# Expert loop of an attention and mixture-of-experts kernel: x and h transposed together, each iteration ending on layer 2, the last tile taken out of the loop

## The reference, cut to what matters

```python
# attention: 4 batches x 8 heads, queries averaged in pairs: 1152 keys, 576 queries, 64 dims
x = attention(q, k, v)                        # [4, 576, 512]
for b in range(B):
    for s in range(S):
        fresh_e = argmax(logits[b, s])        # gate of 8 experts
        e = fresh_e if s == 0 or local_gate[b, s] < 0.5 else prev_e
        p = softmax(logits[b, s])
        h = np.maximum(x[b, s] @ w1[e], 0.0)  # 512 -> 1024
        out[b, s] = p[e] * (h @ w2[e])        # 1024 -> 512
```

## Time and profile before

| | us |
|---|---|
| median of 3 runs | 859.22 |
| lowest and highest run | 855.77 and 859.75 |
| the profiled execution | 858.52 |
| its span, first to last instruction | 856.7 |
| PE busy | 836.5 (98%) |
| DVE busy | 465.8 (54%) |
| ACT busy | 400.5 (47%) |

### The profile page before, as it was taken

One profiled execution on the slowest core, in us unless ns is written; L12 is line 12 of the kernel. 1 busy time (PEld: TensorE's weight loads), 2 busy tenths in 40 slices (PEclk: granted clock), 3 DMA queues, 4 the chain that ended last, 5 costly groups with the idle time before them and its releaser, 6 DMA issues. The chain is left out here.

```text
span 856.7 us, 14360 instructions
## 1 busy us (share of the span) xinstructions
PE 836.5 (98%) x5400; PEld 536.4 (63%) x5401; DVE 465.8 (54%) x669; ACT 400.5 (47%) x572; POOL 332.3 (39%) x323
## 2 busy tenths in 40 slices
PE   6999999999999999999999998999999999999995
PEld 6887877878878788788788774533333333333331
DVE  4676776766767757767777563622332422323322
ACT  4655655655655656565565551324233232242230
POOL 6574375365366357347338310021222221221211
PEclk8999999999999999999999998999999999999997
DMA  7332333242242284332561006576616373110100
GB/s 277 111 91 103 113 118 97 98 140 69 97 147 63 98 81 145 110 132 70 215 214 41 13 18 221 215 248 230 220 37 205 113 273 124 37 32 19 37 24 18
DMA packets 54327, 100.92 MB, mean 118 GB/s; under 512 B 27589, under 2 KB 27589, under 8 KB 54280
## 3 DMA queue, kind: packets, MB, share of 16 engines
q1 hardware_dynamic: 50712, 90.03, 32.1%
q0 software_dynamic: 3568, 10.23, 3.6%
HBM read 90.78 MB, written 9.99 MB: 118 GB/s over the span
## 5 line engine op out<-in xcount | busy, mean ns | idle before, releaser
L844 DVE TENSOR_REDUCE negmax<-psum 128x1 f32<-128x1152 f32 x144 | 195.3, 1357 | 103.4 <-PE psum L518 86.8
L658 ACT ACTIVATE probs<-psum,negmax 128x1152 f32<-128x1152 f32 x128 | 156.6, 1224 | 56.1 <-DVE negmax L844 51.9
L518 PE MATMUL psum<-kstack,qstack 128*128 128x384 f32 x768 | 169.3, 356 | 2.6 <-ACT probs L658 2.2
L543 PE MATMUL psum<-ident,probs 128*128 128x128 f32 x1152 | 160.8, 276 | 3.2 <-ACT probs L658 2.8
L543 PEld LDWEIGHTS psum<-ident,probs 128*128 128x128 f32 x1152 | 134.4, 142 | 15.7 <-issue 6.2
L518 PEld LDWEIGHTS psum<-kstack,qstack 128*128 128x128 f32 x768 | 130.3, 191 | 10.4 <-ACT probs L658 9.6
L1323 PE MATMUL psum<-wbuf,shared 128*64 x288 | 130.1, 605 | 3.8 <-DVE second L1515 3.8
L1325 PE MATMUL psum<-second,shared 128*64 128x512 f32 x288 | 130.1, 605 | 0.0
L653 ACT ACTIVATE pT<-psum 128x512 f32<-128x512 f32 x160 | 95.2, 595 | 69.8 <-PE psum L543 68.8
L1304 PE MATMUL psum<-wbuf,xgT 128*64 x288 | 127.4, 595 | 0.3 <-issue 0.3
L1306 PE MATMUL psum<-second,xgT 128*64 128x512 f32 x288 | 127.4, 595 | 0.0
(11 more groups left out here) (243 smaller groups left out, 977.1 us busy)
## 6 DMA issues: line engine op xcount, KB each, us to landing
wbuf<-in_w SPq DMA_DIRECT2D x64, 512.0 KB, 4.4
qraw<-in_q_t SPq DMA_DIRECT2D x32, 576.0 KB, 4.3
kraw<-in_k_t SPq DMA_DIRECT2D x32, 576.0 KB, 6.2
vraw<-in_v_t SPq DMA_DIRECT2D x16, 576.0 KB, 4.1
x_rows<-x_out SPq DMA_DIRECT2D x32, 128.0 KB, 2.0
second<-in_w SPq DMA_DIRECT2D x8, 512.0 KB, 7.3
x_rows<-x_out SPq DMA_DIRECT2D x32, 16.0 KB
e_rows<-early_rows SPq DMA_DIRECT2D x4, 72.0 KB, 3.8
```

Of the source, the lines that this page charges most:

```text
L518: last = nc.tensor.matmul(dst[:, third, 0:THIRD], qstack[p % 2][:, part, tile_cols(side, i)], kstack[p % 2][:, side, third * THIRD:(third ...
L543: last = nc.tensor.transpose(dst[:, i * P:(i + 1) * P], probs[side][:, i, c * P:(c + 1) * P], ident[:])
L658: nc.scalar.activation(probs[side][:, i, :].rearrange("p (a b) -> p a b", a=3), slot(f, i)[:, :, 0:THIRD], ACT.Exp, bias=negmax[:, p % 2, ...
L844: nc.vector.tensor_reduce(negmax[:, p % 2, col:col + 1], slot(f, i)[:, :, 0:THIRD], AX.XY, ALU.max, negate=True).then_inc(max_ready, 1)
```

## The change

PE's loop body becomes: transpose x of tile t, transpose h of tile t-1, layer 1 of tile t, layer 2 of tile t-1. The loop ends one tile earlier. The last tile is written out behind it, with its layer 1 cut in two around layer 2 of the tile before. The x transposes go to two PSUM banks; ACT saves one half and DVE the other. The h transposes signal after each half, and layer 2 waits for the second half of hT only in its middle. DVE's loop saves hT before y. The number of the last tile is read ahead of the loop, and POOL copies the last tile's row numbers to `dst_last` before it is needed.

```diff
-    src_now, dst_now = sb("src_now", [P, 1], I32), sb("dst_now", [P, 1], I32)
+    src_now, dst_now, dst_last = sb("src_now", [P, 1], I32), sb("dst_now", [P, 1], I32), sb("dst_last", [P, 1], I32)
-    h_ps, hT_ps, xT_ps, y_ps = psum[:, 0:2, :], psum[:, 2:4, :], psum[:, 4, :], psum[:, 5, :]
+    h_ps, hT_ps, xT_ps, y_ps = psum[:, 0:2, :], psum[:, 2:4, :], [psum[:, 4, :], psum[:, 7, :]], psum[:, 5, :]
...
@@ POOL
+        last = tile_count(pool, less=1)
+        nc.gpsimd.tensor_copy(dst_last[:], dst_i[:, bass.ds(last, 1)])
         scatter(tile_count(pool, less=2))
-        scatter(tile_count(pool, less=1))
+        pool.wait_ge(y_last_saved, 1)
+        nc.gpsimd.indirect_dma_start(out=out_rows, out_offset=bass.IndirectOffsetOnAxis(ap=dst_last[:, 0:1], axis=0),
+                                     in_=y[:], in_offset=None, bounds_check=TOK - 1, oob_is_err=False).then_inc(scattered, 16)
         pool.wait_ge(scattered, 16 * count)
+        pool.wait_ge(gathered, 16 * count + 16)
@@ ACT
+        def save_x(t):
+            act.wait_ge(xT_full, t + 1)
+            nc.scalar.activation(xgT[:, 0:DC // 2, :].rearrange("p c d -> p (c d)"), xT_ps[0][:, 0:2 * P], ACT.Copy).then_inc(xT_saved_a, 1)
...
         copy_second1(0, first=True)
-        with act.Fori(0, SLOTS) as t:
-            with act.If(t < count):
+        save_x(0)
+        save_h(0)
+        copy_second1(1)
+        save_x(1)
+        save_hT(0)
+        with act.Fori(1, SLOTS) as t:
+            with act.If(t < last):
                 save_h(t)
                 copy_second1(t + 1)
+                save_x(t + 1)
                 save_hT(t)
+        save_h(last)
+        save_hT(last)
@@ PE
-        def layer1(t, expert):
-            pe.wait_ge(xT_saved, t + 1)
-            pe.wait_ge(w_ready, expert + 1)
-            pe.wait_ge(second1_ready, t + 1)
+        def layer1(t, expert, first=0, end=2 * DC):
+            if first == 0:
+                pe.wait_ge(w_ready, expert + 1)
+                pe.wait_ge(second1_ready, t + 1)
+                pe.wait_ge(xT_saved_a, t + 1)
+                pe.wait_ge(xT_saved_b, t + 1)
...
-            last.then_inc(hT_full, 1)
+                if c % 4 == 3:
+                    last.then_inc(hT_full, 1)
 
         def layer2(t, expert):
+            pe.wait_ge(second2_ready, t + 1)
             pe.wait_ge(hT_saved_a, t + 1)
-            pe.wait_ge(hT_saved_b, t + 1)
-            pe.wait_ge(second2_ready, t + 1)
             for c in range(FC):
+                if c == FC // 2:
+                    pe.wait_ge(hT_saved_b, t + 1)
...
+        pe.wait_ge(early_y_saved, 1)
         transpose_x(0)
         early_layer2(1, 2, 4)
         layer1(0, now)
         early_layer2(1, 4, 8)
-        transpose_x(1)
-        transpose_h(0)
+        prior = tile_count(pe, less=2)
         with pe.Fori(1, SLOTS) as t:
-            with pe.If(t < count):
+            with pe.If(t < last):
                 now, before = experts_of(t)
+                transpose_x(t)
+                transpose_h(t - 1)
                 layer1(t, now)
-                transpose_x(t + 1)
                 layer2(t - 1, before)
-                transpose_h(t)
-        _, before = experts_of(count)
-        layer2(tile_count(pe, less=1), before)
+        now, before = experts_of(last)
+        transpose_x(last)
+        transpose_h(prior)
+        layer1(last, now, 0, 2)
+        layer2(prior, before)
+        layer1(last, now, 2, 2 * DC)
+        transpose_h(last)
+        layer2(last, now)
@@ DVE
         def save_x(t):
             dve.wait_ge(xT_full, t + 1)
-            nc.vector.tensor_copy(xgT[:].rearrange("p c d -> p (c d)"), xT_ps[:, :]).then_inc(xT_saved, 1)
+            nc.vector.tensor_copy(xgT[:, DC // 2:DC, :].rearrange("p c d -> p (c d)"), xT_ps[1][:, 0:2 * P]).then_inc(xT_saved_b, 1)
...
                 save_h(t)
                 save_x(t + 1)
+                save_hT(t)
                 save_y(t - 1)
-                save_hT(t)
                 copy_second2(t)
-        save_y(tile_count(dve, less=1))
+        save_y(tile_count(dve, less=2))
+        copy_second2(last)
+        save_h(last)
+        save_hT(last)
+        save_y(last, saved=y_last_saved)
```

More of the change, by code:

```diff
@@ L1031, in experts @@
     gathered, scattered = sem("gathered"), sem("scattered")
-    xT_full, xT_saved = sem("xT_full"), sem("xT_saved")
+    xT_full, xT_saved_a, xT_saved_b = sem("xT_full"), sem("xT_saved_a"), sem("xT_saved_b")
     h_full, h_saved_a, h_saved_b = sem("h_full"), sem("h_saved_a"), sem("h_saved_b")
     hT_full, hT_saved_a, hT_saved_b = sem("hT_full"), sem("hT_saved_a"), sem("hT_saved_b")
-    y_saved = sem("y_saved")
+    y_saved, y_last_saved = sem("y_saved"), sem("y_last_saved")
     early_xT_full, early_xT_saved = sem("early_xT_full"), sem("early_xT_saved")
@@ L1052, in tile_count @@
     def tile_count(eng, less=0):
-        return eng.value_load(counts[0:1, less:less + 1], min_val=TOK // P - less, max_val=SLOTS - less)
+        return eng.value_load(counts[0:1, less:less + 1], min_val=TOK // P - EARLY - less, max_val=SLOTS - less)
     @block.sync
@@ L1180, in save_h @@
             nc.scalar.activation(h[:, 0:HALF], h_ps[:, 0, :], ACT.Relu).then_inc(h_saved_a, 1)
+        def save_x(t):
+            act.wait_ge(xT_full, t + 1)
+            nc.scalar.activation(xgT[:, 0:DC // 2, :].rearrange("p c d -> p (c d)"), xT_ps[0][:, 0:2 * P], ACT.Copy).then_inc(xT_saved_a, 1)
         def save_hT(t):
-            act.wait_ge(hT_full, t + 1)
+            act.wait_ge(hT_full, 2 * t + 1)
             nc.scalar.activation(hT[:, 0:4, :].rearrange("p c d -> p (c d)"), hT_ps[:, 0, :], ACT.Copy).then_inc(hT_saved_a, 1)
@@ L1198, in _ @@
         act.wait_ge(plan_ready, 1)
-        count = tile_count(act)
+        last = tile_count(act, less=1)
         copy_second1(0, first=True)
-        with act.Fori(0, SLOTS) as t:
-            with act.If(t < count):
+        save_x(0)
[5 more added lines that the diff above has]
+            with act.If(t < last):
                 save_h(t)
                 copy_second1(t + 1)
+                save_x(t + 1)
                 save_hT(t)
+        save_h(last)
+        save_hT(last)
     @block.tensor
@@ L1293, in transpose_x @@
             for c in range(DC):
-                last = nc.tensor.transpose(xT_ps[:, c * P:(c + 1) * P], xg[:, c * P:(c + 1) * P], ident[:])
+                last = nc.tensor.transpose(xT_ps[c // 2][:, c % 2 * P:(c % 2 + 1) * P], xg[:, c * P:(c + 1) * P], ident[:])
             last.then_inc(xT_full, 1)
-        def layer1(t, expert):
-            pe.wait_ge(xT_saved, t + 1)
-            pe.wait_ge(w_ready, expert + 1)
-            pe.wait_ge(second1_ready, t + 1)
[L1301 to L1308, removed]
+        def layer1(t, expert, first=0, end=2 * DC):
[4 more added lines that the diff above has]
+                pe.wait_ge(xT_saved_b, t + 1)
+            for n in range(first, end):
+                half, c = n // DC, n % DC
+                at = c * FF + half * HALF
+                nc.tensor.matmul(h_ps[0:ROWS, half, :], xgT[:, c, 0:ROWS], wbuf[:, bass.ds(weights_at(expert) + at, HALF)],
+                                 start=(c == 0), stop=(c == DC - 1))
+                done = nc.tensor.matmul(h_ps[ROWS:P, half, :], xgT[:, c, ROWS:P], second1[:, at:at + HALF],
+                                        start=(c == 0), stop=(c == DC - 1))
+                if c == DC - 1:
+                    done.then_inc(h_full, 1)
         def transpose_h(t):
@@ L1354, in _ @@
         pe.wait_ge(plan_ready, 1)
-        count = tile_count(pe)
+        last = tile_count(pe, less=1)
         now, _ = experts_of(0)
+        pe.wait_ge(early_y_saved, 1)
         transpose_x(0)
@@ L1496, in save_hT, with save_y @@
         def save_hT(t):
-            dve.wait_ge(hT_full, t + 1)
+            dve.wait_ge(hT_full, 2 * t + 2)
             nc.vector.tensor_copy(hT[:, 4:8, :].rearrange("p c d -> p (c d)"), hT_ps[:, 1, :]).then_inc(hT_saved_b, 1)
-        def save_y(t, first=False):
+        def save_y(t, first=False, saved=y_saved):
             dve.wait_ge(y_done, t + 1)
@@ L1503, in save_y @@
                 dve.wait_ge(scattered, 16 * t)
-            ts(y[:], y_ps[:, :], pslot[:, bass.ds(t, 1)], None, ALU.mult).then_inc(y_saved, 1)
+            ts(y[:], y_ps[:, :], pslot[:, bass.ds(t, 1)], None, ALU.mult).then_inc(saved, 1)
         def copy_second2(t, first=False):
@@ L1533, in _ @@
         copy_second2(1)
-        count = tile_count(dve)
+        last = tile_count(dve, less=1)
         with dve.Fori(2, SLOTS) as t:
-            with dve.If(t < count):
+            with dve.If(t < last):
                 save_h(t)
                 save_x(t + 1)
+                save_hT(t)
                 save_y(t - 1)
-                save_hT(t)
                 copy_second2(t)
-        save_y(tile_count(dve, less=1))
+        save_y(tile_count(dve, less=2))
[3 more added lines that the diff above has]
+        save_y(last, saved=y_last_saved)
```

## The result

The changed kernel takes 850.85 us in the median of 4 runs (850.14 to 851.84); the kernel before took 858.75 beside it (855.77 to 859.75, 4 runs). The ratio is 0.9915 with a 95% interval of 0.9887 to 0.9942. The forecast was 851.7, inside 848.5 to 856.7. The profiled execution took 851.38 and its span is 849.3; the sum had said 851.7 and 849.9.

The account below looks back on a forecast made before the run. PE bounds the kernel from about 556 us. A period of 15.34 us, the last layer 2 at 835.14, an end at 847.28 and 2.6 for the clock give span 849.9, time 851.7; range 848.5 to 856.7.

Parts of the forecast that it names:

- the sum: Whole kernel: the predicted terms added up to a span of 849.9 us and a time of 851.7 us.
- The handovers: PE's loop: one change into transposes and out instead of two, period 15.34 us for 15.64, gain 0.30 per iteration.
- T: Start of the x transposes in an iteration; the prediction counts its times from there, such as layer 1 at T + 1.47.
- The start: First tiles: new wait costs 0, first loop x transposes stay at 569.85, T of tile 2 is 585.17.
- The last x transposes: Tile 17 after the loop: they start at 815.27, from 585.17 plus 15 periods of 15.34 us.
- The stall: Layer 2 of tile 16, behind four pairs: PE idles 2.82 us for DVE's weight copy, restarting at 821.32.
- The clock: Behind the new stall: TensorE's clock falls to 0.50, costing 2.6 us, bounds 0 and about 3.1.
- the clock stays up: Rival at the new stall: no clock fall there, sum 849.1 us; chance 0.17.
- The end: Last layer 2 starts at 835.14, then 12.62 us less 0.48 on the last scatter: end 847.28 before the clock term.
- The real gain of the last tile: Last tile: DVE saves y and copies its second2 weights in about 4 us under the other 12 layer 1 pairs.
- the gain per tile would be eaten by the new wait: Rival in the loop: layer 1 starts at T + 1.82, 0.35 more on 16 tiles, 857.3 us; chance 0.13.
- The slower rival: Loop: ACT's x copy is held behind a weight copy waiting for a load; 865 us at T + 2.3; chance 0.04.

Follow-up runs that it names:

- the experiment with one copy: Changed kernel with x transposed into one PSUM bank and saved by DVE alone in one copy of 512 columns: median 852.96 us, ratio 0.9945.
- the one with h first: Changed kernel with h of the tile before transposed ahead of x in PE's loop: median 865.69 us, ratio 1.009 to the kernel before.
- the second profile: Changed kernel run again with no edit: median 850.01 us in 6 runs, ratio 0.990 to the kernel before.
- where they are read ahead: Changed kernel with the last layer 1 cut after 4 steps and the last tile's experts read before PE's loop: median 848.05 us, ratio 0.9873.
- row numbers late: Changed kernel with the last tile's row numbers copied, and the copy drained, only after y is ready: one run, 850.16 us.
- y first: Changed kernel with DVE's loop saving y before hT again: median 848.31 us, ratio 0.9889 to the kernel before.
- The experiment with the old ending: Changed kernel with the last layer 1 uncut and DVE's last saves in the order h, y, hT, second2: median 850.91 us, ratio 0.9931.
- the cut after four steps: Changed kernel with the last tile's layer 1 cut after 4 steps (8 pairs) instead of 2 (4 pairs): median 846.74 us, ratio 0.9881.
- the old loop with the new ending: Changed kernel with the old order in PE's and DVE's loops, keeping the last tile outside and its layer 1 cut: median 853.89 us, ratio 0.9937.

## Why the prediction was right, step by step

**The handovers.** The mechanism and the size are right. The period was forecast at 15.34 and is 15.36; layer 1 starts at T + 1.47 (632.79 - 631.32), as worked out. The copy of 256 columns takes 0.42 on DVE and 0.38 on ACT, as read off between the rows of other widths. Only one term of this step was wrong, and it did not matter: the restart after the save of x is 0.29 and not 0.36. x is saved at T + 1.12 (632.02 + 0.42), so the save would let layer 1 start at T + 1.41, and PE's own transposes, not the copy, set the 1.47. The 0.29 comes from the experiment with one copy, and the one with h first shows that their cover is what the order lives on.

**The start.** The x transposes of tiles 0 and 1 are at 557.09 and 569.92, 0.1 later than before, and T of tile 2 is 585.25 for a forecast of 585.17. The new wait for `early_y_saved` was put at 0 and may have cost the 0.1: from the end of the save it waits for (555.39 + 0.75) to the transposes it is 0.95 us, and 1.00 in the second profile, where the kernel before, which does not wait for it, has 0.81 and 0.87.

**The last x transposes** came at 816.14, 0.87 us later than the 815.27 of the sum. Of this, 0.47 is the one thing that the prediction passed over: PE's sequencer leaves the loop and reads the last experts in front of them. (From the last pair at 815.14 it is 1.00, and 0.53 where they are read ahead; the profile's own column has 0.41.) I had looked at such a lag in the steady loop only, as a rival, and costed the way out of the loop at nothing. The rest is the 0.08 of the start and 0.02 on each of 15 tiles.

**The stall.** Its place and its releaser were forecast. The size was 2.82, the wait shown is 2.07 (2.24 between the end of the fourth pair and the restart). DVE's copy ended at T + 5.22, not T + 5.69, and the restart behind it took 0.26, not 0.36. The 0.39 between DVE's last save and its weight copy, taken from the old order, does not occur at this place: the copy starts at 819.00 and y ends at 819.06. That row belonged to the old sequence of instructions, and the term was mis-sized by it. It is not enough that y is the last save. In front of the next weight copy of the same profile DVE saves y alone, after a wait, and the gap is there with 0.32 (831.40 to 831.72); with y saved before hT it is 0.27. What decides it was not tried.

**The clock.** It fell in the profiled execution, as forecast, but for 1.7 us and not 2.6. In another execution it did not fall. The prediction gave "the clock stays up" a chance of 0.17, which is too little for a thing that varies from one execution to the next: of the six profiles with a stall of 1.9 to 2.1 us, it fell in three (the changed kernel's first, h first, row numbers late) and stayed up in three (the changed kernel's second, one copy, y first).

**The end.** The last layer 2 starts at 837.02; the sum with its clock term put it at 835.14 + 2.6 = 837.74. From there to the end of the span it takes 12.28 for a forecast of 12.14. So there are errors of +0.9 (the last x transposes late), -0.6 (the restart behind the stall at T + 5.48, not T + 6.05) and -0.9 (the clock), and the small ones cancel each other; 0.6 us is left on the span. That the total is nearer than its terms is luck. The last scatter's 0.48 was near: from the end of y to the issue it is 0.81, which is 0.55 less than before.

**The real gain of the last tile.** The prediction saw it in the weight copy for the last tile, which now runs under 12 pairs. The experiment with the old ending puts the cut at only 0.9 us with the clock up. By start times PE is idle there for 3.84 us between the h transposes and the last layer 2 (834.86 to 838.70). In the changed kernel it is idle for 2.24 at the new place and for 0.68 between the h transposes and the last layer 2 (837.02 - 835.48, less the 0.86 of the transposes), where the saves of h and hT now have no cover. The loop order gives 4.0 to 5.8.

**The rivals.** That the gain per tile would be eaten by the new wait is refuted by the period. The slower rival (ACT's x copy behind a late weight load) did not occur: ACT's copy starts at the same 632.02 as DVE's, and at the same time in all 18 tiles.

## What to carry to other kernels

Here TensorE lost 0.3 us per tile to a second change into transposes and out again, so it paid to put all transposes of an iteration together, but only in the order in which the result that is needed first has the other transposes as its cover. The end of a stall that another engine sets does not move with the bound engine's own work: put as much of the bound engine's work before it as the rest of the chain allows, here eight pairs and not four. Behind a loop with a fixed bound and a run-time condition, read ahead what the code after it needs, since the sequencer arrives there late.

## What the runs showed of the hardware

- Idle time alone did not decide whether TensorE's granted clock fell. At the end stall it fell after 3.81, 3.82 and 3.94 us of waiting, and stayed at 1.00 after 3.61. The wait behind the attention, 2.9 us in twelve profiles and 3.60 in that of the cut after four steps, brought it down in all 13. With one and the same program and a wait of 2.07 us it fell in one profile and stayed in the other. The fall cost 1.7 us after the short stalls and 2.6 to 3.0 after the long ones.
- The first 557 us or so differ between executions by up to 5 us in where the expert loop starts (554.6 to 559.6), about as much as single runs of one kernel differ. Stretches taken from a common event told differences of 0.5 us that the medians did not.
- In the changed kernel POOL's copy of row numbers takes 0.97 us where it took 0.18. It starts 0.3 us after DVE's weight copy has begun, and the scatter's issue takes 1.03 where it took about 2.2. Where a POOL instruction starts while DVE's weight copy runs, its end follows DVE: the scatter issues that start then end 0.12 us after the weight copy, in the kernel before (841.25 and 841.12), in the changed one (834.20 and 834.08) and in the old loop with the new ending (826.58 and 826.46). So POOL seems to wait for DVE here, and that was not tried by an edit.
